# Expert tail: the early half folded ahead of the late half's value products, output tiles turned two ahead in four banks, the last tile in two halves

## The reference, cut to what matters

```python
def _moe2_ref(x, w_gate, wq, wk, wv, wo) -> np.ndarray:   # B, S, D = 2, 768, 512; E = 4; Hd = 64
    ...
    for e in range(E):
        q = x @ wq[e]
        k = x @ wk[e]
        v = x @ wv[e]
        scores = scale * (q @ k.transpose(0, 2, 1))        # causal
        ...
        a = np.exp(scores)
        a /= a.sum(-1, keepdims=True) + 1e-09
        ye = a @ v @ wo[e]
        for kk in range(K):
            mask = topk[:, :, kk] == e
            out += mask[..., None] * w[:, :, kk:kk + 1] * ye
```

## Time and profile before

| | us |
|---|---|
| median of three runs | 727.9 |
| the three runs | 727.56, 727.9, 729.34 |
| profiled execution, its own time | 728.61 |
| its span, from the first to the last instruction | 726.7 |
| PE busy | 690.4 (95%) |
| ACT busy | 391.9 (54%) |
| DVE busy | 385.0 (53%) |
| POOL busy | 298.1 (41%) |

### The profile page before, as it was taken

The page is one execution under the profiler, slowest core; times in us unless marked ns, Lnnn a source line. Parts: engine busy times, 40 slices in busy tenths (PEclk is TensorE's granted clock), DMA queues, the critical chain, the costliest instruction groups (busy, mean ns, idle before and its releaser), DMA issues. The chain is left out here.

```text
span 726.7 us, 11879 instructions
## 1 busy us (share of the span) xinstructions
PE 690.4 (95%) x3796; PEld 541.9 (75%) x3796; DVE 385.0 (53%) x828; ACT 391.9 (54%) x797; POOL 298.1 (41%) x260
## 2 busy tenths in 40 slices
PE   5899999999999998999999999999999989999986
PEld 4667666766776756888888888888888978888864
DVE  4888888888888856111112111211112757886571
ACT  3777776677777655323333333333333656676663
POOL 6655655655565201544534454445443012332110
PEclk9999999999999999999999999999999999999999
DMA  4112211111220493200000000000000000000102
GB/s 155 45 55 78 85 55 54 54 54 55 90 71 11 93 336 103 58 0 0 0 0 0 0 0 0 0 0 0 0 0 10 21 0 2 0 1 30 59 2 87
DMA packets 25196, 30.28 MB, mean 42 GB/s; under 512 B 8784, under 2 KB 19152, under 8 KB 25168
## 3 DMA queue, kind: packets, MB, share of 16 engines
q1 hardware_dynamic: 25168, 29.93, 12.9%
HBM read 26.78 MB, written 3.15 MB: 41 GB/s over the span
## 5 line engine op out<-in xcount | busy, mean ns | idle before, releaser
L885 DVE SCALAR_TENSOR_TENSOR hid_l<-psT,hid_h 128x512 fp32r<-128x512 f32 x48 | 33.2, 691 | 212.1 <-ACT hid_h L861 212.1
L909 POOL TENSOR_TENSOR w_l<-w_raw,w_h 128x512 fp32r<-128x512 f32 x48 | 61.9, 1290 | 134.7 <-ACT w_h L852 134.7
L409 ACT ACTIVATE probs<-psS,scale_bias 128x768 f32<-128x768 f32 x96 | 95.1, 991 | 36.9 <-DVE scale_bias L490 36.4
L480 DVE TENSOR_REDUCE negmax<-psS 128x1 f32<-128x768 f32 x96 | 91.5, 953 | 9.5 <-PE psS L317 5.1
L330 PE MATMUL psT<-ident,probs 128*128 128x128 f32 x576 | 84.1, 277 | 3.8 <-ACT pt L418 1.8
L330 PEld LDWEIGHTS psT<-ident,probs 128*128 128x128 f32 x576 | 66.4, 141 | 21.3 <-issue 9.6
L852 ACT ACTIVATE w_h<-w_raw 128x512 fp32r (+1 forms) x48 | 30.3, 631 | 95.2 <-PE psS L818 95.2
L316 PE MATMUL psS<-k_hh,q_lh 128*128 128x384 f32 x192 | 73.8, 385 | 4.2 <-ACT probs L409 2.0
L807 PE MATMUL psT<-x_h,w_h 128*128 x192 | 74.8, 390 | 0.7 <-DVEq L877 0.7
L807 PE MATMUL psT<-x_h,w_l 128*128 x192 | 74.8, 390 | 0.0
L807 PE MATMUL psT<-x_l,w_h 128*128 x192 | 74.8, 389 | 0.0
(11 more groups left out here) (184 smaller groups left out, 1453.3 us busy)
## 6 DMA issues: line engine op xcount, KB each, us to landing
raw<-qk SPq DMA_DIRECT2D x16, 768.0 KB, 4.7
w_raw<-w SPq DMA_DIRECT2D x16, 256.0 KB, 6.8
w_raw<-w SPq DMA_DIRECT2D x4, 1024.0 KB, 8.8
raw_v<-v_n SPq DMA_DIRECT2D x16, 192.0 KB, 2.3
out<-y_out SPq DMA_DIRECT2D x12, 256.0 KB, 2.0
wvg_raw<-wv SPq DMA_DIRECT2D x4, 128.0 KB, 3.1
wqk_raw<-wq SPq DMA_DIRECT2D x4, 128.0 KB, 2.8
wqk_raw<-wk SPq DMA_DIRECT2D x4, 128.0 KB, 2.7
```

What stands on the lines that cost most here:

```text
L409: nc.scalar.activation(probs[j % 3][:].rearrange("p (c n) -> p c n", c=2), psS[:, score_slot(p, j), :, 0:HALF], ACT.Exp, bias=scale_bias[: ...
L480: nc.vector.tensor_reduce(negmax[:, p, j:j + 1], psS[:, score_slot(p, j), :, 0:HALF], AXIS.XY, ALU.max, negate=True).then_inc(rowmax_ready, 1)
L909: nc.gpsimd.tensor_tensor(w2_l[s][:].rearrange("p a b -> p (a b)"), w2_raw[:, f, :], w2_h[s][:].rearrange("p a b -> p (a b)").bitcast(F32) ...
```

## The change

In the tail the generic steps are replaced by a list of its own for each engine. `steps` ends with head 7, and then:

- PE runs `fold(7, 0)` between pieces 1 and 2 of the value products, turns tiles 0 and 1, runs `fold(7, 1)`, and then outputs tile n and turns tile n + 2, for n = 0 to 5.
- `turn_mixed` waits for one half less (`- (t < 4)`) where the tile is in the early half. This holds for batch 0 too.
- DVE runs `low_mixed` of tile 0 between the two `add_halves` of head 7. ACT splits tile n + 2 ahead of copying result n.
- Batch 1's results use four banks, `psS[:, t % 2, t // 2 % 2, :]`, and there are four `y_out` buffers (`YB`) for both batches.
- The last tile is multiplied in two halves of 256 columns, in two banks; each half has its own copy on ACT and its own DMA.

The diff, cut to its core:

```diff
+    YB = 4
-        y = [sb(f"y_out{s}", [P, C]) for s in range(2)]
+        y = [sb(f"y_out{s}", [P, C]) for s in range(YB)]
...
-        steps = [(h, j) for h in range(HEADS_E + 2) for j in range(QT)] + [(HEADS_E + 2, 0), (HEADS_E + 2, 1)]
+        steps = [(h, j) for h in range(HEADS_E) for j in range(QT)]
+        END = HEADS_E
...
+        late_tiles = [(1, t) for t in range(QT)]
...
-            return psS[:, t % 2, 0, :] if b == 1 else psT[:, place["y", b, t] % 2, :]
+            return psS[:, t % 2, t // 2 % 2, :] if b == 1 else psT[:, place["y", b, t] % 2, :]
+
+        def y_halves(tile):
+
+            if tile != late_tiles[-1]:
+                return [(y_bank(*tile), slice(0, C))]
+            return [(psS[:, 1, 0, 0:C // 2], slice(0, C // 2)), (psS[:, 0, 1, 0:C // 2], slice(C // 2, C))]
...
-                    pe.wait_ge(norm_done, 2 * (b + 1) * E)
+                    pe.wait_ge(norm_done, 2 * (b + 1) * E - (t < 4))
...
-                    elif t < 2:
+                    elif t < 4:
                         pe.wait_ge(exp_done, 6 * HEADS_E)
                     else:
-                        pe.wait_ge(y_copied, count[use] - 2)
+                        pe.wait_ge(y_copied, count[use] - 4 + (tile == late_tiles[-1]))
                     pe.wait_ge(low_done, count[("m", b, t)])
-                    for c in range(2):
-                        for m, (x, w) in enumerate(((mixed_h, wo_h), (mixed_h, wo_l), (mixed_l, wo_h))):
-                            last = nc.tensor.matmul(y_bank(b, t), x[t % 2][:, c, :], w[:, c, :],
-                                                    start=(c == 0 and m == 0), stop=(c == 1 and m == 2))
+                    halves = y_halves(tile)
+                    for to, cols in halves:
+                        for c in range(2):
+                            for m, (x, w) in enumerate(((mixed_h, wo_h), (mixed_h, wo_l), (mixed_l, wo_h))):
+                                last = nc.tensor.matmul(to, x[t % 2][:, c, :], w[:, c, cols],
+                                                        start=(c == 0 and m == 0), stop=(c == 1 and m == 2))
+                        if to is not halves[-1][0]:
+                            last.then_inc(last_half_ready, 1)
                     last.then_inc(y_ready, 1)
...
+                transposes(END - 1, 4)
+                value_products(END - 1, 0)
+                transposes(END - 1, 5)
+                value_products(END - 1, 1)
+                fold(END - 1, 0)
+                value_products(END - 1, 2)
+                value_products(END - 1, 3)
+                turn_mixed(late_tiles[0])
+                turn_mixed(late_tiles[1])
+                fold(END - 1, 1)
+                for n, tile in enumerate(late_tiles):
+                    output(tile)
+                    if n + 2 < QT:
+                        turn_mixed(late_tiles[n + 2])
...
+                high(END - 1, 5)
+                copy_output(END - 1, 0)
+                copy_output(END - 1, 1)
+                split_mixed(late_tiles[0])
+                split_mixed(late_tiles[1])
+                for n, tile in enumerate(late_tiles):
+                    if n + 2 < QT:
+                        split_mixed(late_tiles[n + 2])
+                    copy_y(tile)
...
+                low(END - 1, 5)
+                add_halves(END - 1, 0)
+                low_mixed(late_tiles[0])
+                add_halves(END - 1, 1)
+                for tile in late_tiles[1:]:
+                    low_mixed(tile)
```

More of the change, by code:

```diff
@@ L1158, in out_tile @@
         def out_tile(h, j, back=0):
[L1160 to L1164, removed]
-        steps = [(h, j) for h in range(HEADS_E + 2) for j in range(QT)] + [(HEADS_E + 2, 0), (HEADS_E + 2, 1)]
+            n = (h - E - 1) * QT + j - 1 - back
+            return (0, n) if 0 <= n < QT else None
+        steps = [(h, j) for h in range(HEADS_E) for j in range(QT)]
+        END = HEADS_E
         uses, late_uses = [], []
+        late_tiles = [(1, t) for t in range(QT)]
         in_step = {0: [("t", 1, 4), ("m",), ("y",)],
@@ L1177, in expert_attention @@
                  5: [("t", 0, 3), ("y",), ("m",)]}
-        for h, j in steps:
+        for h, j in steps + [(END, 0), (END, 1)]:
             for kind, *of in in_step[j]:
@@ L1182, in expert_attention @@
                 elif kind != "t" and out_tile(h, j, kind == "y"):
-                    b, n = out_tile(h, j, kind == "y")
-                    (late_uses if kind == "y" and b == 1 else uses).append((kind, b, n))
+                    uses.append((kind, *out_tile(h, j, kind == "y")))
+        for tile in late_tiles:
+            uses.append(("m", *tile))
+            late_uses.append(("y", *tile))
         place = {u: n for n, u in enumerate(uses)}
@@ L1297, in turn_mixed, with output @@
                     last.then_inc(t_ready, 1)
-                def output(h, j):
-                    tile = out_tile(h, j, 1)
+                def output(tile):
                     if tile is None:
@@ L1323, in _ @@
                         value_products(h - 1, 0)
[L1324 to L1325 removed]
+                        turn_mixed(out_tile(h, j))
+                        output(out_tile(h, j, 1))
                     if j == 1:
@@ L1416, in copy_y @@
                     use = ("y", b, n)
+                    i = b * QT + n
+                    if i >= YB:
+                        act.wait_ge(y_sent[i % YB], 16 * (i // YB))
+                    halves = y_halves(tile)
+                    if len(halves) == 2:
+                        at, cols = halves[0]
+                        act.wait_ge(last_half_ready, 1)
+                        nc.scalar.activation(y[i % YB][:, cols], at, ACT.Copy).then_inc(last_half_copied, 1)
+                    at, cols = halves[-1]
                     act.wait_ge(y_ready, count[use])
-                    if count[use] > 2:
-                        act.wait_ge(y_sent[n % 2], 16 * ((count[use] - 1) // 2))
-                    nc.scalar.activation(y[n % 2][:], y_bank(b, n), ACT.Copy).then_inc(y_copied, 1)
+                    nc.scalar.activation(y[i % YB][:, cols], at, ACT.Copy).then_inc(y_copied, 1)
                 for h, j in steps:
                     if j == 0:
-                        split_mixed(h, j)
+                        split_mixed(out_tile(h, j))
                         exp(h, 0)
-                        copy_y(h, j)
+                        copy_y(out_tile(h, j, 1))
                         high(h - 1, 5)
                     if j == 1:
-                        split_mixed(h, j)
+                        split_mixed(out_tile(h, j))
                         exp(h, 1)
-                        copy_y(h, j)
+                        copy_y(out_tile(h, j, 1))
                     if j == 2:
@@ L1560, in _ @@
                         route.make_gates(1)
+                add_halves(END - 2, 0)
+                low(END - 1, 4)
+                add_halves(END - 2, 1)
+                row_factors(END - 1)
+                low(END - 1, 5)
[4 more added lines that the diff above has]
+                    low_mixed(tile)
             @block.gpsimd
@@ L1595, in _ @@
                 for i in range(NT):
-                    sp.wait_ge(y_copied, i + 1)
                     b, t = i // QT, i % QT
-                    sp.dma_start(out[b, t * P:(t + 1) * P, :], y[i % 2][:]).then_inc(y_sent[i % 2], 16)
-                for s in range(2):
-                    sp.wait_ge(y_sent[s], 16 * NT // 2)
+                    halves = y_halves((b, t))
+                    for at, cols in halves:
+                        if cols.stop < C:
+                            sp.wait_ge(last_half_copied, 1)
+                        else:
+                            sp.wait_ge(y_copied, i + 1)
+                        sp.dma_start(out[b, t * P:(t + 1) * P, cols], y[i % YB][:, cols]).then_inc(y_sent[i % YB], 16)
+                for s in range(YB):
+                    sp.wait_ge(y_sent[s], 16 * (NT // YB + (s == (NT - 1) % YB)))
 def build(nc, qk_2, v_n, proj_2, U, V, w1, w2, w_gate, wq, wk, wv, wo, out):
```

64 lines of the change are left out of this document (31 added, 33 removed).

## The result

The changed kernel takes 724.02 us (median of seven runs, 722.84 to 725.98), the kernel before 727.9 (also seven runs, 727.56 to 729.34). The ratio is 0.9937, with a 95% interval of 0.9924 to 0.9951: faster by 0.63%, or 3.9 us by the medians.

What follows compares the result with a forecast made beforehand. It took the tail's chain of waits across engines, where PE idles, as the bound. Gains of 1.87 + 1.18 + 0.22 + 0.2 = 3.5 us off the 727.9 median gave 724.4 us, range 723.3 to 726.0.

Steps and rivals of the forecast that it cites:

- The range: Whole kernel's time: 723.3 to 726.0 us, from term bounds of 724.1 and 725.5 plus half a microsecond either side.
- Early fold: Start of the tail: folding the early half ahead of late value products moves tile 0's turn earlier, gaining 1.87 us.
- the 0.40 us of transposes: PE's early fold delays the late value products by 0.40 us, hidden before tile 0's turn with 0.09 us of cover.
- Two ahead: Output stream: turning two tiles ahead removes the stall before tile 4 and a little before tile 3, gaining 1.18 us.
- The last tile: End of the stream: two halves cost PE nothing, shorten the last copy by 0.22 us and the DMA by 0.2.
- The DMA: Last output DMA: half the bytes save 0.2 us, the middle between 0.4 and nothing.
- No cost in batch 0: Batch 0: the lowered wait and four output buffers cost nothing and gain nothing.
- The sum: All terms together: 1.87 + 1.18 + 0.22 + 0.2 = 3.5 us of gain.
- Rival D: PE's granted clock falls to 1.2 GHz in the tail; each output costs 1.4 us, all six give 732.8; chance 0.02.

Runs made afterwards that it cites:

- Both halves waited for: Changed kernel with the early fold kept, but the turns waiting for both halves and the late fold ahead of them: first output at 6.40 us, tail 19.96 us.
- with fills: Changed kernel and kernel before, each with PE's two pauses filled by unused matmuls (the kernel before also in its tail waits): 722.18 us and 725.54 us.
- the first experiment: Changed kernel with the early fold, the turns' lowered wait and the order of DVE's two additions put back as before: tail 20.20 us.
- with the pieces: Changed kernel with the two pauses filled, and head 7's early half processed in two pieces of two query tiles: 721.42 us, ratio to before 0.9907.
- with the late fold: Changed kernel with early fold, lowered wait and DVE's addition order undone, the two pauses and PE's two tail waits filled: 724.18 us, tail 18.57 us.

## Why the prediction was right, point by point

The range of 723.3 to 726.0 holds the 724.02, and the direction is the forecast one.

- *Early fold, 1.87 us.* Measured 1.85. PE's turn waited for POOL's first multiplication, as forecast, and the 0.40 us of transposes were hidden, with 0.19 us of cover instead of 0.09. "Both halves waited for" showed that the early fold without the lowered wait brings 0.08 of it.
- *Two ahead, 1.18 us.* Measured 1.20. That the releaser named in rows 5 was the wrong one is shown by the stall that came back with four banks and stayed away with two. I gave the banks a part ("take `y_copied` off the path"); they have none. The sum is right, but its wording is not: there was no stall before tile 3, whose output started 1.54 us after that of tile 2; tile 4's came 2.88 us after tile 3's, and the rest of the 1.18 is small differences of a few hundredths.
- *The last tile.* PE's part 0 (12 x 0.12 us), the copy 0.22, as forecast. The DMA is the mis-sized term: 0.2 as the middle of 0 and 0.4, and 0.29 measured in the profiles, 0.33 against the kernel with the last tile whole. The formula of the Trainium skill (DMA: Bandwidth & Descriptors, "Anatomy of one DMA") gives an estimated 0.30 for this difference. But the section has it for DMAs that GpSimd issues, and those here are issued by SP, which the prediction passed over. Its fixed 2.0 us is not borne out by them, as a DMA of 128 KB landed in 1.8 us here.
- *No cost in batch 0.* Nothing here speaks against it: with fills, the marks of the changed kernel and of the one before lie 0.23 us apart, and 0.27 us are there at 42 us already, long ahead of batch 0's outputs.
- *The sum* was 3.5 for a tail that shrank by 3.57. The medians moved by 3.9. The profiled execution is another matter: its span was to be near 723.2 and was 720.7. Of these 2.5 us 2.43 lie ahead of the mark, where the forecast had nothing, because it took over the level of an execution with two stretches at half clock.
- *The range.* By its own terms it should start at 724.1 - 0.5 = 723.6, not at 723.3. The median lies inside either way.
- *Rival D* was judged on a wrong reading. I wrote that the clock had stayed up in all 40 slices; a slice with a digit 9 can hide 3 us at half clock, and the very profile held two such stretches. The mechanism is real, but in the tail only kernels with the long waits showed it: in the first experiment waits of 1.45 and 0.81 us with four transposes between them stood ahead of the fall, and the kernel before has the same two waits, though its profile shows no fall there. None of the nine profiles with the changed start of the tail shows one while PE works. The price was too high as well: I had 8.4 us for six outputs at half clock, and a stretch lasted 3.4 us and cost 1.6.

What the clock does to the totals is best seen by runs of equal mean clock. Runs of the kernel before, beside the experiments, and of the changed kernel:

| mean clock | before, us | after, us |
|---|---|---|
| 1.000 | none unfilled | 722.84 |
| 0.997 and 0.998 | 727.4 to 728.0 | 723.58 to 724.14 |
| 0.995 | 728.6 to 729.3 | 725.98 |
| 0.993 | 730.1 to 730.3 | none |

A step from row to row is one stretch at half clock, 1.2 to 2.0 us by the medians of the rows. Within the two rows that both kernels share the change brings between 2.6 and 4.4 us, so nothing contradicts 3.5. In the profiled executions 0.998 was one stretch and 0.995 two; read so, of 22 such runs of before nine had one, ten had two and three had three; of the seven of after one had none, five one and one two. Three stretches need a third place, and the tail is the only one in which any profile shows it; that it was the tail in those three runs is inferred, since only the profiled executions were looked into. Whether the change makes such runs rarer stays open, with seven runs after. The medians don't need it. The four faster of the seven runs of before (727.56 to 727.9, clock not recorded) lie at the level of one stretch, and their median is 727.72; the five such runs of after have 724.02. That makes 3.7 us, and 727.9 is the highest of those four.

## What to carry to other kernels

At the end of a kernel, where nothing runs beside it, look at what each step really needs: here the turn of an output tile waited for a half of the data in which it has no part, and moving the work ahead and lowering one wait together were worth 1.8 us, while moving the work without lowering the wait was worth 0.1. Run each producer two steps ahead of its consumer, and test a name in the column of releasers by taking that cause away before buying banks for it. Compare two profiles from a mark that the change doesn't touch, and scan the granted clock in windows of 1 us first, or a fall of the clock that has nothing to do with the change is booked on it.

## What was not expected of the hardware

- At a pause of PE of 2.3 to 2.6 us, its granted clock is in some executions halved for 3.3 to 3.4 us and in others not. It costs 1.2 to 1.6 us each time. With matmuls that fill all but 0.8 us of each pause, none of 20 runs showed it: their mean clock was 0.999 or 1.000 (five runs of the changed kernel, five of the one before, four with the pieces, six with the late fold), and the scatter of the changed kernel went from 3.1 us to 0.3.
- The fall can come while PE still idles (at 274.0 in the profile of before, 0.6 us before it resumed) or when it is already busy again: 1.5 us after in the same profile, 0.8 us after the stream had begun in the first experiment.
- A DMA of half the bytes and the same 128 rows ended the kernel 0.29 to 0.33 us sooner; the 256 KB moved for 0.8 us, so it is a little less than half of that.
